# Attention tiles of a fused kernel: logits and turning of x in 64x64 blocks, tiles loaded in halves, weights loaded beside the first tiles

## The chip, the cores and the metric

The kernel runs on one core of one Trainium2 chip. Time is device microseconds (us) of one execution; three executions of the kernel before are shown below. Engines are TensorE (PE), VectorE (DVE), ScalarE (ACT), GpSimd (POOL) and SyncE (SP), which issues all the DMAs.

## The reference, cut to what matters

```python
# q, k, v: (8 batches, 8 heads, 576, 64)
scores = (q @ k.transpose(0, 1, 3, 2)) / sqrt(64)
Dmat[h] = where(i >= j, gamma[h] ** (i - j), 0)          # decay by distance
x = (scores * Dmat) @ v                                  # -> (4608 tokens, 512)
logits = x @ phi                                         # phi: 512 x 32 slots
d = exp(logits - logits.max(0)); d /= d.sum(0) + 1e-9    # over the tokens
slot_in = d.T @ x                                        # 32 x 512
slot_out[e] = relu(slot_in[e] @ w1[e]) @ w2[e]           # 8 experts, 4 slots each
c = exp(logits - logits.max(1)); c /= c.sum(1) + 1e-9    # over the slots
y = c @ slot_out
out = (((y @ fw1) * (y @ fw2)) @ fw3) @ w_out
```

## The kernel before

The 4608 tokens are 36 tiles of 128, in four groups of nine tiles (two batches each). Attention is computed by chunks of 64 positions with a running state: for each tile TensorE makes the scores inside the chunks (`scores`, L648), the products k and v that update the state (`update`, L661), the output through the states (`through_states`, L676) and through the masked scores (`through_scores`, L693, in two phases of 16 pairs). All of these are matmuls on 64x64 blocks of the array, four of which lie side by side. The result leaves in turned form (channels on the partitions); VectorE multiplies it by the decay and writes `x_t` (`scale_x`, L1249).

From `x_t` two things are made. `logits` (L711) multiplies by `phi` in the 128x32 shape, with `phi` as weights; the result, slots on the partitions, goes to the bank `RAW`, and ScalarE copies it to `logits_raw` (L1016). `turn_x` (L705) turns `x_t` by four 128x128 transposes into the bank `X_NAT`, and ScalarE copies it to `x_nat` (L1007). After each group VectorE and ScalarE compute maxima, exp and the combine weights `c_nat` (one step of it in each of the next tiles), and `dispatch` (L727, L732, 128x32 shape) sums exp times x over the group; ScalarE's `copy_sums` (L1050) takes the sum out of the same bank.

TensorE's order for tile n is written out in `step`: scores and update of n+1, a dispatch if one is due, logits of n-2, states of n, phase 0 of n, turn of n-1, phase 1 of n. TensorE runs it in a loop of nine passes with four steps as its body; parts that only some passes need (a dispatch, the logits of a tile before the first) stand in the body behind a branch. The other engines' orders are unrolled. In float32 one matmul of the program shows as two pairs of a weight load and a matmul.

SP issues everything from one queue, in a fixed order: the constants, tiles 0 and 1 in two halves each, tiles 2 and 3, weight unit 0, then tile by tile, with units 1 to 5 at tiles 4, 5 and 8 and four fold transfers behind tiles 10, 11, 14 and 15 (`FOLD_AT`). A tile is 1 MB with q turned, k turned, k, v; it is loaded when the tile four places before it is out (`out_ready`), as there are four places. A weight unit and a fold transfer are 1 MB too. POOL scales v as soon as the tile is there (`scale_v`, L561), and the scores of a tile wait for it (`v_ready`). Units 6 to 35 and two more folds wait for the last tiles or for the use of earlier units.

After the tiles TensorE makes the product of the last two weight matrices (`fold_part`, L794) in turns with the 36 expert and feature units (L809, L909), then pair features (L931) and the final product (L991).

Of the kernel before, what the change touches and what calls it, by code (L numbers as in the profile page):

```python
# [55 lines left out]
FOLD_AT = (10, 11, 14, 15)  # L56
# [24 lines left out]
def build(nc, pkg, consts, phi, units, fold_w, out, c_rows):  # L81
    ctx = ExitStack()
    with ctx:
# [39 lines left out]
        logits_raw = place("logits_raw", [P, 2, TILES * SLOTS])  # L123
# [101 lines left out]
        OUT_T, UPDATE, X_NAT, RAW = 2, 4, 6, 7  # L225
        STATE, LOGITS, MISC = 4, 6, 7

# [8 lines left out]
        tile_loaded = [sem(f"tile_loaded{i}") for i in range(SLOTS_IN)]  # L236
        first_loaded = [sem(f"first_loaded{i}") for i in range(2)]
# [10 lines left out]
        x_nat_ready = sem("x_nat_ready")  # L248
        logits_ready = sem("logits_ready")
# [6 lines left out]
        exp_ready = sem("exp_ready")  # L256
        raw_turned = sem("raw_turned")
        exp_nat_ready = sem("exp_nat_ready")
        sums_ready = sem("sums_ready")
        sums_copied = sem("sums_copied")  # L260
# [68 lines left out]
        def q_t(n):  # L329
            return tile_sb(n)[:, 0:D].rearrange("p (a n) -> p a n", a=PAIRS)  # L330

        def k_t(n):
            return tile_sb(n)[:, D:2 * D].rearrange("p (a n) -> p a n", a=PAIRS)

        def k_nat(n):
            return tile_sb(n)[:, 2 * D:3 * D]
# [101 lines left out]
        def _(sp):  # L438
            def load_tile(n):
# [16 lines left out]
            def load_first(t, half):  # L456

                lo, hi = 2 * D * half, 2 * D * (half + 1)
                sp.dma_start(pkg_sb[:, t, lo:hi], pkg[t].rearrange("(p c) -> p c", p=P)[:, lo:hi]
                             ).then_inc(tile_loaded[t] if half else first_loaded[t], 16)  # L460

            sp.dma_start(const_sb[:, 0:C_LATE], consts[:, 0:C_LATE]).then_inc(const_loaded, 16)
            for t in range(2):
                load_first(t, 1)
                load_first(t, 0)
# [4 lines left out]
            load_tile(2)  # L470
            load_tile(3)
# [17 lines left out]
            for u in range(6, UNITS):  # L489
# [3 lines left out]
                if u == 9:  # L493

                    sp.wait_ge(x_turned, NTILES)
# [143 lines left out]
        def _(pe):  # L639
# [44 lines left out]
            def through_scores(r, phase):  # L684

                for a in range(PAIRS):
                    for half in range(2):
# [10 lines left out]
                        elif phase == 1:  # L698
                            last.then_inc(phase_done, -1)
                        elif half == 0:  # L700
                            last.then_inc(x_t_ready if a == 0 else logits_copied, -1)

            def turn_x(r):
                for a in range(PAIRS):
                    last = nc.tensor.transpose(psum[:, X_NAT, P * a:P * (a + 1)], x_t[:, r % 2, a, :], ident)  # L705
                last.then_inc(x_turned, 1)

            def logits(r):
                for a in range(PAIRS):
                    for j in range(SUBS):  # L710
                        last = mm(psum[SLOTS * j:SLOTS * (j + 1), RAW, 0:SLOTS], phi_sb[:, a, :],  # L711
                                  x_t[:, r % 2, a, SLOTS * j:SLOTS * (j + 1)],
                                  start=(a == 0), stop=(a == PAIRS - 1))
                        if a == PAIRS - 1:
                            last.then_inc(logits_ready, 1)

            def dispatch(g):

                pe.wait_ge(exp_nat_ready, g + 1)
                pe.wait_ge(x_nat_ready, NTILES if g == GROUPS - 1 else dispatched_at(g) - 1)  # L720
# [20 lines left out]
            def step(i, r):  # L741
# [4 lines left out]
                else:  # L746
                    with pe.If(i < NTILES // SLOTS_IN - 1):
                        next_scores(after)
                for g in range(GROUPS - 1):
# [3 lines left out]
                if r > 1:  # L753
                    logits(two_before)
                else:
                    with pe.If(i > 0):
                        logits(two_before)

                pe.wait_ge(x_t_ready, 1)
                through_states(r)  # L760
                pe.wait_ge(logits_copied, 1)
                through_scores(r, 0)
                if r > 0:
                    turn_x(before)
                else:
                    with pe.If(i > 0):
                        turn_x(before)
# [3 lines left out]
            pe.wait_ge(first_loaded[0], 16)  # L771
# [3 lines left out]
            pe.wait_ge(first_loaded[1], 16)  # L775
# [78 lines left out]

            logits(SLOTS_IN - 2)
# [3 lines left out]
            logits(SLOTS_IN - 1)  # L859
            turn_x(SLOTS_IN - 1)  # L860
            fold(5)
# [20 lines left out]
            pe.wait_ge(x_nat_ready, NTILES)  # L882
# [119 lines left out]
        def _(act):  # L1002
            copy = nc.scalar.copy

            def copy_x(n):
                act.wait_ge(x_turned, n + 1)
                copy(x_nat[:, n % NAT_RING, :], psum[:, X_NAT, :]).then_inc(x_nat_ready, 1)  # L1007

            def copy_logits(n):
                g, t = divmod(n, TILES)  # L1010
                act.wait_ge(logits_ready, SUBS * (n + 1))
                if g >= 2 and t == 0:

                    act.wait_ge(raw_turned, g - 1)
                    act.wait_ge(exp_ready, g - 1)
# [561 lines left out]
```

## Time and profile before

| | us |
|---|---|
| median of 3 runs | 393.22 (392.13 to 396.33) |
| the profiled execution | 394.4 |
| its span, first to last instruction | 392.6 |
| TensorE matmuls busy | 358.9 (91%) |
| mean granted clock of TensorE | 0.969 |
| DMA | 104.77 MB, 267 GB/s over the span |

A row of a timeline begins with its start and its duration in us, then engine, line, operation, what it writes and reads, its shape and how many were merged; brackets give the engine's idle time before it and what ended that. TensorE's matmuls are pipelined: a group's duration reaches into the next group, so the time that a group takes is read from start to start.

### The profile page before, as it was taken

The page shows a single profiled execution, that of the slowest core. Times are in us where ns is not written, and L with a number is a line of the kernel's source. Part 1 is how long each engine was busy: PE and PEld are TensorE (multiplying, and loading weights), DVE is VectorE, ACT ScalarE, POOL GpSimd, SP SyncE. Part 2 cuts the span into 40 slices and gives each one's busy share as a digit, 9 for nine tenths or more (in the row PEclk, how much of TensorE's full clock was granted, in tenths as well). Part 3 has the DMA queues.
Part 4 walks back from the last instruction along what each step waited for, and adds up shares of the span by engine and source line. Part 5 has one row for each costly group of instructions (what it writes and reads, how often), then busy time and mean ns, then how long its engine had stood idle before and what let it go on. Part 6 is the DMA issues. An engine that isn't in the chain of part 4 may idle for free. (4 is left out here: it accounts for less than half of the span.)

```text
span 392.6 us, 16090 instructions
## 1 busy us (share of the span) xinstructions
PE 358.9 (91%) x7123; PEld 278.2 (71%) x7123; DVE 167.5 (43%) x329; ACT 125.2 (32%) x275; POOL 161.9 (41%) x155
## 2 busy tenths in 40 slices
PE   2683987898999999999999999899999999999996
PEld 1573876777878887774656555468878888888885
DVE  1321454556757765573013000699853323233320
ACT  1000121321433342222324220532734444434442
POOL 2521222322443542133546451298954554554530
PEclk9856799999999999999999999999999999999999
DMA  7898499897887886879999996057226655556222
GB/s 262 351 387 341 149 398 426 337 374 250 312 308 240 313 310 231 314 294 411 427 425 427 425 428 273 0 92 237 76 88 228 230 189 188 190 179 235 114 107 107
DMA packets 25914, 104.77 MB, mean 267 GB/s; under 512 B 2660, under 2 KB 5284, under 8 KB 16164
## 3 DMA queue, kind: packets, MB, share of 16 engines
q1 hardware_dynamic: 25892, 104.47, 71.1%
q8 instruction: 14, 0.23, 0.2%
q14 instruction: 8, 0.07, 0.0%
HBM read 94.14 MB, written 10.32 MB: 266 GB/s over the span
## 5 line engine op out<-in xcount | busy, mean ns | idle before, releaser
L561 POOL TENSOR_TENSOR pkg_sb<-pkg_sb,const_sb 128x512 f32<-128x512 f32 x36 | 37.5, 1042 | 106.4 <-DMA pkg_sb<-in_tiles 106.4
L623 POOL TENSOR_TENSOR feat<-c_sb 128x512 f32<-128x512 f32 x45 | 56.9, 1275 | 46.2 <-PE psum L991 44.3
L991 PE MATMUL psum<-m_hi,feat_hi 128*128 128x512 f32 x144 | 56.1, 390 | 0.3 <-DVE m_lo L1480 0.3
L991 PE MATMUL psum<-m_lo,feat_hi 128*128 128x512 f32 x144 | 56.0, 389 | 0.0
L991 PE MATMUL psum<-m_hi,feat_lo 128*128 128x512 f32 x144 | 56.0, 389 | 0.0
L428 DVE TENSOR_TENSOR feat_lo<-feat,feat_hi 128x512 fp32r<-128x512 f32 x34 | 27.2, 801 | 62.2 <-ACT feat_hi L1149 61.0
L1249 DVE TENSOR_TENSOR x_t<-psum,x_decay 128x512 f32<-128x512 f32 x36 | 24.9, 691 | 40.9 <-PE psum L693 40.9
L1007 ACT COPY x_nat<-psum 128x512 f32<-128x512 f32 x36 | 21.1, 586 | 65.8 <-PE psum L705 65.8
L648 PE MATMUL psum<-pkg_sb 64*64 64x64 f32 x1152 | 26.9, 234 | 16.2 <-POOL pkg_sb L561 7.3
L693 PE MATMUL psum<-weights_t,pkg_sb 64*64 64x64 f32 x1152 | 35.3, 238 | 5.7 <-issue 5.5
L1149 ACT CAST feat_hi<-feat 128x512 fp32r<-128x512 f32 x45 | 27.9, 623 | 39.0 <-POOL feat L623 39.0
L588 POOL TENSOR_TENSOR w_lo<-fold_raw,w_hi 128x512 fp32r<-128x512 f32 x14 | 18.2, 1298 | 45.1 <-ACT wo_hi L1066 45.0
L648 PEld LDWEIGHTS psum<-pkg_sb 64*64 64x64 f32 x1152 | 23.4, 146 | 17.7 <-issue 17.5
L693 PEld LDWEIGHTS psum<-weights_t,pkg_sb 64*64 64x64 f32 x1152 | 26.2, 141 | 12.9 <-issue 12.6
L991 PEld LDWEIGHTS psum<-m_hi,feat_hi 128*128 128x128 f32 x144 | 27.0, 188 | 6.2 <-issue 0.7
L1207 DVE TENSOR_TENSOR weights_t<-psum,const_sb 128x512 f32<-128x512 f32 x36 | 24.7, 686 | 15.6 <-PE psum L648 14.9
L991 PEld LDWEIGHTS psum<-m_hi,feat_lo 128*128 128x128 f32 x144 | 27.0, 188 | 5.6
L991 PEld LDWEIGHTS psum<-m_lo,feat_hi 128*128 128x128 f32 x144 | 27.0, 188 | 5.6
L1230 DVE TENSOR_TENSOR state_sb<-psum,state_sb 128x256 f32<-128x256 f32 x56 | 23.5, 420 | 14.7 <-PE psum L676 12.4
L676 PE MATMUL psum<-pkg_sb,state_sb 64*64 64x64 f32 x1152 | 26.7, 234 | 2.1 <-issue 1.6
L1193 ACT COPY out_sb<-psum 128x512 f32<-128x512 f32 x36 | 21.2, 589 | 21.5 <-PE psum L991 19.5
L661 PE MATMUL psum<-pkg_sb 64*64 64x64 f32 x1152 | 27.3, 234 | 0.7 <-issue 0.7
(138 smaller groups left out, 569.0 us busy)
## 6 DMA issues: line engine op xcount, KB each, us to landing
pkg_sb<-in_tiles SPq DMA_DIRECT2D x34, 1024.0 KB, 4.9
unit_a<-in_units SPq DMA_DIRECT2D x16, 1024.0 KB, 13.8
c_sb<-c_rows SPq DMA_DIRECT2D x45, 256.0 KB
unit_x<-in_units SPq DMA_DIRECT2D x9, 1024.0 KB, 14.1
out<-out_sb SPq DMA_DIRECT2D x36, 256.0 KB, 2.0
fold_raw<-in_fold SPq DMA_DIRECT2D x6, 1024.0 KB, 9.3
unit_y<-in_units SPq DMA_DIRECT2D x5, 1024.0 KB, 12.3
unit_n<-in_units SPq DMA_DIRECT2D x4, 1024.0 KB, 12.2
```

The source lines that it names most:

```text
L428: engine.tensor_tensor(feat_lo[:, k, :], feat[:, k, :], feat_hi[:, k, :].bitcast(F32), ALU.subtract).then_inc(done, 1)
L561: nc.gpsimd.tensor_tensor(v_nat(n).rearrange("p (h d) -> p h d", h=HEADS), v_nat(n).rearrange("p (h d) -> p h d", h=HEADS), decay.unsqueez ...
L623: nc.gpsimd.tensor_tensor(feat[:, k, :], c_sb[:, s, x, :], c_sb[:, s, y, :], ALU.mult).then_inc(feat_ready, 1)
L648: last = mm(psum[cols, odd, HD * a:HD * (a + 1)], k_t(r)[rows, a, cols], q_t(r)[rows, a, cols], start=True, stop=True)
L661: last = mm(psum[HD * odd:HD * (odd + 1), UPDATE + half, HD * a:HD * (a + 1)], k_nat(r)[rows, cols], v_nat(r)[rows, cols], start=True, sto ...
L676: last = mm(out_of(a, odd, half), state_sb[rows, (2 * r + half) % STATES_IN, a, :], q_t(r)[rows, a, HD * half:HD * (half + 1)], start=(hal ...
L693: last = mm(out_of(a, odd, half), v_nat(r)[rows, HD * h:HD * (h + 1)], weights_t[rows, r % 2, odd, HD * a:HD * (a + 1)], start=False, stop ...
L991: last = mm(psum[:, OUT + b, :], x, y, start=(at == 0 and m == 0), stop=(at == 4 and m == 2))
L1149: copy(feat_hi[:, ORDER[at], :], feat[:, ORDER[at], :]).then_inc(feat_hi_ready, 1)
L1207: tt(weights_t[:, n % 2, :, :].rearrange("p k (a n) -> p k a n", a=PAIRS), psum[:, 0:2, 0:D // 2].rearrange("p k (a n) -> p k a n", a=PAIR ...
L1230: tt(to, new, state_sb[:, c % STATES_IN, :, :].rearrange("p a n -> p (a n)"), ALU.add).then_inc(done, 1)
L1249: tt(x_t[:, n % 2, :, :].rearrange("p (k b) n -> p k (b n)", k=2), psum[:, OUT_T:OUT_T + 2, 0:D // 2], x_decay[:, :, n0:n0 + P].rearrange( ...
```

## The change

- `logits` becomes 16 matmuls on 64x64 blocks with `x_t` as weights and `phi` as the moving side: tokens come on the partitions, and the sum over the two halves of the channels comes in two parts, in two banks. ScalarE copies both parts (`logit_parts`); VectorE adds them once for tiles 0 to 7 of a group and once for tile 8 and transposes the sum into `logits_raw` (`add_parts`). The transpose that made `comb` is gone, as the sum already has that form.
- `turn_x` becomes 16 matmuls on 64x64 blocks with the identity as the moving side, in the same two banks as the logits. So logits wait for ScalarE's copy of x (`x_copied`), and the turn waits for the copy of the logits (`logits_copied`).
- `dispatch` moves behind the states of its step; a new semaphore, `dispatch_free`, tells that both banks are free; ScalarE copies the sums after the logits.
- A tile's layout is k turned, k, q turned, v; the first half is loaded once the scores and update of the tile four before are done, the second once that tile is out, and the keys of tile n+1 are issued ahead of q and v of tile n.
- Weight units 0 and 1 are issued behind tile 3, units 2, 3 and 4 at tile 4, unit 5 at tile 5; the four folds behind tiles 6, 7, 9 and 11.

```diff
-FOLD_AT = (10, 11, 14, 15)
+FOLD_AT = (6, 7, 9, 11)
-        OUT_T, UPDATE, X_NAT, RAW = 2, 4, 6, 7
+        OUT_T, UPDATE, X_NAT = 2, 4, 6
+        LOGITS_AT = D // 2
...
+            def load_keys(n):
+                if n >= SLOTS_IN:
+                    for i in range(2):
+                        sp.wait_ge(scores_ready[i], 2 * (n - SLOTS_IN + 1))
+                        sp.wait_ge(update_ready[i], 2 * (n - SLOTS_IN + 1))
+                sp.dma_start(tile_sb(n)[:, 0:2 * D], pkg[n].rearrange("(p c) -> p c", p=P)[:, 0:2 * D]
+                             ).then_inc(keys_loaded[place_of(n)], 16)
+            def load_q_v(n):
+                if n >= SLOTS_IN:
                     sp.wait_ge(out_ready, QUARTERS * (n - SLOTS_IN + 1))
-                sp.dma_start(tile_sb(n), pkg[n].rearrange("(p c) -> p c", p=P)).then_inc(tile_loaded[place_of(n)], 16)
+                sp.dma_start(tile_sb(n)[:, 2 * D:4 * D], pkg[n].rearrange("(p c) -> p c", p=P)[:, 2 * D:4 * D]
+                             ).then_inc(q_v_loaded[place_of(n)], 16)
...
+            for t in range(2, SLOTS_IN):
+                load_keys(t)
+                load_q_v(t)
             load_first_unit(0)
+            load_first_unit(1)
+            load_keys(SLOTS_IN)
             for n in range(SLOTS_IN, NTILES):
-                load_tile(n)
+                if n < NTILES - 1:
+                    load_keys(n + 1)
+                if n == SLOTS_IN:
+                    load_first_unit(2)
+                    load_first_unit(3)
+                load_q_v(n)
                 if n < SLOTS_IN + 2:
-                    load_first_unit(2 * n - 7)
-                    load_first_unit(2 * n - 6)
-                elif n == 8:
-                    load_first_unit(5)
+                    load_first_unit(n)
                 elif n in FOLD_AT:
...
             def scale_v(n):
-                pool.wait_ge(tile_loaded[place_of(n)], (n // SLOTS_IN + 1) * 16)
+                pool.wait_ge(q_v_loaded[place_of(n)], (n // SLOTS_IN + 1) * 16)
+                if n >= 2:
+                    pool.wait_ge(keys_loaded[place_of(n)], (n // SLOTS_IN + 1) * 16)
...
-            def turn_x(r):
+            def turn_x(r, consumes=True):
                 for a in range(PAIRS):
-                    last = nc.tensor.transpose(psum[:, X_NAT, P * a:P * (a + 1)], x_t[:, r % 2, a, :], ident)
-                last.then_inc(x_turned, 1)
+                    for odd in range(2):
+                        rows = slice(HD * odd, HD * (odd + 1))
+                        for half in range(2):
+                            cols = slice(HD * half, HD * (half + 1))
+                            last = mm(psum[cols, X_NAT + odd, HD * a:HD * (a + 1)], x_t[rows, r % 2, a, cols],
+                                      ident[rows, rows], start=True, stop=True)
+                            if (a, odd, half) == (0, 0, 0) and consumes:
+                                last.then_inc(logits_copied, -1)
+                            if a == PAIRS - 1:
+                                last.then_inc(x_turned, 1)
-            def logits(r):
+            def logits(r, consumes=True):
                 for a in range(PAIRS):
-                    for j in range(SUBS):
-                        last = mm(psum[SLOTS * j:SLOTS * (j + 1), RAW, 0:SLOTS], phi_sb[:, a, :],
-                                  x_t[:, r % 2, a, SLOTS * j:SLOTS * (j + 1)],
-                                  start=(a == 0), stop=(a == PAIRS - 1))
+                    for odd in range(2):
+                        rows = slice(HD * odd, HD * (odd + 1))
+                        for half in range(2):
+                            cols = slice(HD * half, HD * (half + 1))
+                            last = mm(psum[cols, X_NAT + odd, LOGITS_AT:LOGITS_AT + SLOTS], x_t[rows, r % 2, a, cols],
+                                      phi_sb[rows, a, :], start=(a == 0), stop=(a == PAIRS - 1))
...
+                if r > 1:
+                    pe.wait_ge(x_copied, 1)
+                    logits(two_before)
...
+                pe.wait_ge(x_t_ready, 1)
+                through_states(r)
                 for g in range(GROUPS - 1):
                     if dispatched_at(g) % SLOTS_IN == r:
                         with pe.If(i == dispatched_at(g) // SLOTS_IN):
                             dispatch(g)
...
                 through_scores(r, 0)
                 if r > 0:
+                    pe.wait_ge(logits_copied, 1)
                     turn_x(before)
...
+            def add_parts(g, last):
+                lo, hi = (SLOTS * (TILES - 1), SLOTS * TILES) if last else (0, SLOTS * (TILES - 1))
+                nat = comb[:, :, :].rearrange("p t s -> p (t s)")[:, lo:hi]
+                dve.wait_ge(group_copied, 2 * g + 1 + last)
+                if g > 0 and not last:
+                    dve.wait_ge(c_ready, g)
+                    dve.wait_ge(exp_ready, g)
+                tt(nat, logit_parts[:, 0, lo:hi], logit_parts[:, 1, lo:hi], ALU.add).then_inc(parts_added, 1)
+                dve.wait_ge(parts_added, 2 * g + 1 + last)
+                nc.vector.transpose(logits_raw[:, lo:hi], nat).then_inc(raw_turned, 1)
```

## Rows read from the trace of the kernel before

**Rows 1.** The page's 40 slices of 9.8 us: clock (tenths) and DMA rate.
```profile
PEclk9856799999999999999999999999999999999999
...
GB/s 262 351 387 341 149 398 426 337 374 250 312 308 240 313 310 231 314 294 411 427 425 427 425 428 273 0 92 237 76 88 228 230 189 188 190 179 235 114 107 107
```
**Rows 2.** Busy time by stretches: length, each engine, clock, DMA share, GB/s.
```profile
0.00:56.50 56.50, 36.71 (x1308) 32.16 (x1308) 18.18 (x35) 6.46 (x14) 13.83 (x18) 0.79 0.82 314
56.50:110.80 54.30, 46.83 (x2181) 40.16 (x2184) 31.26 (x64) 14.74 (x47) 15.62 (x15) 1.00 0.89 339
110.80:165.50 54.70, 53.70 (x2464) 45.17 (x2456) 35.70 (x76) 18.63 (x56) 19.75 (x18) 1.00 0.80 282
165.50:246.90 81.40, 81.40 (x574) 48.41 (x559) 16.88 (x40) 22.04 (x44) 33.45 (x26) 1.00 0.92 381
```
**Rows 3.** Timeline of VectorE: the products x_t of tiles 7, 20, 35.
```profile
56.51 0.69 DVE L1249 TENSOR_TENSOR x_t<-psum,x_decay 128x512 f32<-128x512 f32 x1 [1.08 <-PE psum L693]
...
110.83 0.69 DVE L1249 TENSOR_TENSOR x_t<-psum,x_decay 128x512 f32<-128x512 f32 x1 [1.11 <-PE psum L693]
...
165.49 0.69 DVE L1249 TENSOR_TENSOR x_t<-psum,x_decay 128x512 f32<-128x512 f32 x1 [1.89 <-PE psum L693]
```
**Rows 4.** Timeline of TensorE's matmuls: one step.
```profile
110.17 0.46 PE L693 MATMUL psum<-weights_t,pkg_sb 64*64 64x64 f32 x16
110.45 0.68 PE L648 MATMUL psum<-pkg_sb 64*64 64x64 f32 x32
110.91 0.68 PE L661 MATMUL psum<-pkg_sb 64*64 64x64 f32 x32
111.60 0.48 PE L711 MATMUL psum<-x_t,phi_sb 128*32 128x32 f32 x32
112.02 0.69 PE L676 MATMUL psum<-pkg_sb,state_sb 64*64 64x64 f32 x32
112.59 0.46 PE L693 MATMUL psum<-weights_t,pkg_sb 64*64 64x64 f32 x16
112.98 0.66 PE L705 MATMUL psum<-const_sb,x_t 128*128 128x128 f32 x4
113.56 0.46 PE L693 MATMUL psum<-weights_t,pkg_sb 64*64 64x64 f32 x16
```
**Rows 5.** Timeline of TensorE: nine transposes in a run.
```profile
251.72 1.15 PE L841 MATMUL psum<-const_sb,c_nat 128*128 128x128 f32 x9
```
**Rows 6.** Timeline of TensorE: a dispatch, and the group behind it.
```profile
114.93 1.92 PE L727 MATMUL psum<-x_nat,exp_nat 128*32 128x512 f32 x16
...
116.89 0.56 PE L711 MATMUL psum<-x_t,phi_sb 128*32 128x32 f32 x32
```
**Rows 7.** Timeline of TensorE: the loop's first pass, around its holes.
```profile
16.93 0.58 PE L693 MATMUL psum<-weights_t,pkg_sb 64*64 64x64 f32 x10 [2.98 <-issue]
...
32.94 0.34 PE L693 MATMUL psum<-weights_t,pkg_sb 64*64 64x64 f32 x8 [2.52 <-issue]
...
34.65 0.65 PE L711 MATMUL psum<-x_t,phi_sb 128*32 128x32 f32 x30
38.68 0.31 PE L711 MATMUL psum<-x_t,phi_sb 128*32 128x32 f32 x2 [3.39 <-issue]
```
**Rows 8.** The page's DMA queues: packets, MB, share.
```profile
q8 instruction: 14, 0.23, 0.2%
```
**Rows 9.** Who waited for whom, 56.5 to 110.8 us: total, times, longest.
```profile
PE psum L648 <- POOL pkg_sb L561: 7.3, 6, 1.5
```
**Rows 10.** The page's DMA issues: count, KB each, us to landing.
```profile
pkg_sb<-in_tiles SPq DMA_DIRECT2D x34, 1024.0 KB, 4.9
...
out<-out_sb SPq DMA_DIRECT2D x36, 256.0 KB, 2.0
```
**Rows 11.** Groups of instructions: count, busy us, mean ns, idle before, releaser.
```profile
L561 POOL TENSOR_TENSOR pkg_sb<-pkg_sb,const_sb 128x512 f32<-128x512 f32 x36 | 37.5, 1042 | 106.4 <-DMA pkg_sb<-in_tiles 106.4
...
L1007 ACT COPY x_nat<-psum 128x512 f32<-128x512 f32 x36 | 21.1, 586 | 65.8 <-PE psum L705 65.8
```

More of the change, by code:

```diff
@@ L235, in build @@
         fold_late_loaded = [sem(f"fold_late_loaded{j}") for j in range(FT // 4)]
-        tile_loaded = [sem(f"tile_loaded{i}") for i in range(SLOTS_IN)]
-        first_loaded = [sem(f"first_loaded{i}") for i in range(2)]
+        keys_loaded = [sem(f"keys_loaded{i}") for i in range(SLOTS_IN)]
+        q_v_loaded = [sem(f"q_v_loaded{i}") for i in range(SLOTS_IN)]
         v_ready = sem("v_ready")
@@ L699, in through_scores @@
                             last.then_inc(phase_done, -1)
-                        elif half == 0:
-                            last.then_inc(x_t_ready if a == 0 else logits_copied, -1)
-            def turn_x(r):
+                        elif (a, half) == (0, 0):
+                            last.then_inc(x_t_ready, -1)
+            def turn_x(r, consumes=True):
                 for a in range(PAIRS):
-                    last = nc.tensor.transpose(psum[:, X_NAT, P * a:P * (a + 1)], x_t[:, r % 2, a, :], ident)
-                last.then_inc(x_turned, 1)
@@ new lines, in logits @@
+            def logits(r, consumes=True):
+                for a in range(PAIRS):
+                    for odd in range(2):
[4 more added lines that the diff above has]
+                                      phi_sb[rows, a, :], start=(a == 0), stop=(a == PAIRS - 1))
+                            if (a, odd, half) == (0, 0, 0) and consumes:
+                                last.then_inc(x_copied, -1)
+                            if a == PAIRS - 1:
+                                last.then_inc(logits_ready, 1)
@@ L717, in dispatch @@
             def dispatch(g):
                 pe.wait_ge(exp_nat_ready, g + 1)
-                pe.wait_ge(x_nat_ready, NTILES if g == GROUPS - 1 else dispatched_at(g) - 1)
+                if g == GROUPS - 1:
+                    pe.wait_ge(x_nat_ready, 1)
+                else:
+                    pe.wait_ge(dispatch_free, g + 1)
                 def nat(t):
@@ L748, in step @@
                         next_scores(after)
+                if r > 1:
+                    pe.wait_ge(x_copied, 1)
+                    logits(two_before)
+                else:
+                    with pe.If(i > 0):
+                        pe.wait_ge(x_copied, 1)
+                        logits(two_before)
+                pe.wait_ge(x_t_ready, 1)
+                through_states(r)
                 for g in range(GROUPS - 1):
@@ L858, in _ @@
             pe.wait_ge(x_t_ready, 1)
-            logits(SLOTS_IN - 1)
+            logits(SLOTS_IN - 1, False)
+            fold(1)
+            pe.wait_ge(group_copied, 2 * GROUPS)
             turn_x(SLOTS_IN - 1)
-            fold(5)
+            fold(4)
             dispatch(GROUPS - 1)
@@ L1005, in copy_x @@
             def copy_x(n):
-                act.wait_ge(x_turned, n + 1)
-                copy(x_nat[:, n % NAT_RING, :], psum[:, X_NAT, :]).then_inc(x_nat_ready, 1)
+                act.wait_ge(x_turned, QUARTERS * (n + 1))
+                copy(x_nat[:, n % NAT_RING, :].rearrange("p (a k d) -> p k a d", a=PAIRS, k=2),
+                     psum[:, X_NAT:X_NAT + 2, 0:D // 2].rearrange("p k (a d) -> p k a d", a=PAIRS)
+                     ).then_inc(x_nat_ready if n == NTILES - 1 else x_copied, 1)
             def copy_logits(n):
@@ L1011, in copy_logits @@
                 act.wait_ge(logits_ready, SUBS * (n + 1))
-                if g >= 2 and t == 0:
-                    act.wait_ge(raw_turned, g - 1)
-                    act.wait_ge(exp_ready, g - 1)
-                copy(logits_raw[:, g % 2, SLOTS * t:SLOTS * (t + 1)], psum[:, RAW, 0:SLOTS]
-                     ).then_inc(group_copied if n == NTILES - 1 else logits_copied, 1)
-                if t == TILES - 1 and n < NTILES - 1:
+                if g > 0 and t in (0, TILES - 1):
+                    act.wait_ge(parts_added, 2 * g - (1 if t == 0 else 0))
+                copy(logit_parts[:, :, SLOTS * t:SLOTS * (t + 1)], psum[:, X_NAT:X_NAT + 2, LOGITS_AT:LOGITS_AT + SLOTS]
+                     ).then_inc(group_copied if n == NTILES - 1 else
+                                dispatch_free if n + 2 in [dispatched_at(i) for i in range(GROUPS - 1)] else
+                                logits_copied, 1)
+                if t >= TILES - 2 and n < NTILES - 1:
                     copy(mark[:, :], const_sb[0:1, 0:1]).then_inc(group_copied, 1)
@@ L1085, in relu_hidden @@
                                          ACT.Relu).then_inc(hid_ready, 1)
-            act.sem_inc(logits_copied, 2)
+            act.sem_inc(logits_copied, 1)
             for n in range(1, NTILES):
                 g, t = divmod(n, TILES)
-                if g > 0 and t == 7:
+                if g > 0 and t == 6:
                     exp_combine(g - 1)
+                if n > 1:
+                    copy_logits(n - 2)
                 if g > 0 and n == dispatched_at(g - 1):
                     copy_sums(g - 1)
-                if n > 1:
-                    copy_logits(n - 2)
                 copy_x(n - 1)
```

74 lines of the change are left out of this document (30 added, 44 removed).

## Prediction

> **What bounds the kernel now.** I read the page's slices first: in the first eighth the granted clock falls to 0.5, later it stays at full [rows 1]. So I cut the span by stages [rows 2]. Up to 165.5 us the 36 tiles of attention run; from there TensorE computes folds and expert units, idle nowhere up to 246.9 [rows 2], and then the final product. The change lies in the first stage. The rest is taken to move along unchanged: all 30 later weight units and two folds still wait for the last tiles, and TensorE has no hole behind them that earlier data could fill.
>
> Within the tile stage three parts have different limits; the marks are the products x_t of tiles 7, 20 and 35 [rows 3]. To 56.5 us TensorE is busy 36.7 us, and its longest holes are put down to "issue" [rows 2, 7]. From there to tile 20 it is idle 7.5 of 54.3 us, nearly all of it (7.3) behind the scaling of v, which itself waited for a transfer [rows 2, 9]. From tile 20 to 35 it is idle 1.0 of 54.7 us: the bare order of TensorE's work is the limit. Less two dispatches of 2.2 us (below) that is 50.3 / 15 = 3.36 us a tile.
>
> **Switching of shapes, steady tile.** A step of TensorE lasts 3.39 us, from one phase 1 (L693) to the next [rows 4]. The starts give its parts: phase 1 0.28, scores 0.46, update 0.69, logits (128x32) 0.42, states 0.57, phase 0 0.39, turn (128x128) 0.58. Scores, update and states are each 32 equal pairs of weight load and matmul in 64x64 shape, and 0.46 is what they take with no other shape beside them: update pays 0.23 and states 0.11 for the switch; phase 0, half as many pairs, pays 0.39 - 0.23 = 0.16. The new turn is 32 such pairs, 0.46 where four whole-width transposes and their switch took 0.58; a run of nine of those takes 1.15, some 0.11 each beside the 0.27 of the last [rows 5]. The new logits, 64x64 weights with 32 columns moving, are a form that no row has. They lie between 0.33 (now, less some 0.1 for the switch) and 0.46 (64 columns moving); I take 0.46, since their weights are as wide as those of scores. The step becomes 0.28 + 5 x 0.46 + 0.23 = 2.81: 0.58 less, or 0.71 at the lower end.
>
> **What comes near when a tile is that short.** Loads: a tile is issued when the tile four before is out, lands 4.9 us later, is scaled in 1.04 and some 0.15, and its output is ready 0.4 and two steps after that [rows 3, 10, 11]: 4.9 + 1.2 + 0.4 + 2 x 3.36 = 13.2 against 4 x 3.36 = 13.4. So whole loads are nearly late already, and at 2.81 they would be (12.1 against 11.2). For the half with q and v I interpolate between the 256 KB store (2.0) and the 1 MB load (4.9): 3.0, and 3.0 + 1.6 + 5.6 = 10.2 is in time. At the top end, 4.9, halving gains nothing. The keys' half goes out at its update; scale_v now waits for it too, but it had been sent a good half step earlier. SP is one queue in which the keys of n+1 stand ahead of q and v of n; their condition, update of n-3, is met early in the very step at whose end tile n-4 is out, so they hold nothing up. Bandwidth: 1 MB at the 426 GB/s of full slices is 2.46 us [rows 1], 88% of 2.81. The Trainium skill ("DMA: Bandwidth & Descriptors", Anatomy of one DMA) gives 2.0 us and bytes / 436e3 for a transfer on another issuing path and advises 1 MiB or more: 3.2 us for a half, an estimate. By it the loop would be 10.4, still in time.
>
> ScalarE: banks 6 and 7 now hold x and logits both, so logits wait for copy_x and the turn for copy_logits. A consumer starts 0.20 after the group that it waits for ends (110.83 against 110.17 + 0.46) [rows 3, 4]. From the turn's start 0.68 + 0.20 + 0.59 + 0.1 = 1.57 to the next logits, where TensorE arrives after 0.46 + 0.28 + 0.92 = 1.66; from logits to turn about 1.0 against 1.15 [rows 4, 11]. Behind copy_x ScalarE has four small moves and exp_t queued in one tile of nine; with exp_t taken as long as copy_x the turn waits some 0.4 there. VectorE gets one add and one transpose of 288 columns more a group, less the old transpose, each below the 0.69 of x_t's 512 [rows 3]: under 0.1 a tile, and it is busy 35.7 of 54.7 us [rows 2]. For all of this I allow 0.14 a tile: gain 0.44. Ends: 0 (the handshake takes all) and 0.71.
>
> **Dispatch.** It costs 116.89 - 114.93 = 1.96 us and some 0.2 for switches [rows 6]. It is moved behind states, between two 64x64 groups: one switch more (0.1 to 0.2). And copy_sums, a copy like copy_x (0.59), with 0.3 before and 0.1 behind it, now stands between it and the turn with phase 0 (0.23) as its only cover; before, logits, states and phase 0 hid it. I put 1.0 on each of three dispatches; between 0.2 and 1.5.
>
> **First pass of the loop.** There are five holes by "issue", of 2.98, 1.63, 0.72, 2.52 and 3.39 us, 11.2 in all ([rows 7]: the first and the last two). They lie evenly in the program. From the hole before 32.94 to that before 38.68 there are 8 + 30 pairs, 64 of scores and update between them, and 24 of a dispatch that is jumped over, 126; the others, counted from the start with 64 pairs ahead of the loop, stand at 218, 344, 470 and 596. The page has 14 transfers of the kind "instruction" with 0.23 MB, 16.4 KB each [rows 8]: this is code arriving, a block for each 126 pairs. The turn has 28 pairs more in each of four steps, so the body grows from 728 to 840 pairs and contains one block more. I add a mean hole, 2.2 (0.7 to 3.4). Against it stand eight shorter steps up to tile 7, near 0.5 each: -4. Units 1 to 5 and two folds move ahead into DMA time that is free there (share 0.82) [rows 2]. The second half of tile 4 is then queued behind units 2 and 3, up to 8 us later; its scores ran only behind the hole that ended at 32.94 [rows 7], so this costs 0, or 3 if the queue is longer. Sum -1.8.
>
> **Sum.** To tile 7: -1.8. To tile 20: 13 x -0.44 = -5.7, one dispatch +1.0, and of 7.5 us idle some 3.5 go, since only two folds (9 and 11) are still loaded between those tiles, where a unit and four folds of 2.46 us stood: -8.2. To tile 35: 15 x -0.44 + 2.0 = -4.6. Tail: the last group's add and turn for its last tile, two small operations with their waits, come into the chain from logits over exp_t to the last dispatch, whose cover of folds is used up already: +0.6. In all -14.0: the profiled run's 394.4 (span 392.6 and 1.8 around it) becomes 380.4; the median shown is 1.2 below that run, so 379.
>
> **Rivals.**
> A. Code that has to come back. At the loop's later returns no such hole is seen (TensorE idle 1.0 us over three of them) [rows 2]: the blocks up to pair 792, where the body ends (64 + 728), stay in place. Blocks end at pair 92, 218, ... 722, 848. So the body now reaches from the first block (64 is below 92) into the seventh; at 904 it enters the eighth. If the place for code is then full, the block fetched next displaces the one with the loop's head, and each of eight returns waits for code. Nothing hides that, so it costs at least the longest hole, 3.4: 27 us, of which the idle time behind transfers takes back 4. 380 + 23 = 403, and up to 418, as beside holes of that size the clock stood at 0.5 [rows 1, 7]. From 1.8 us a return on this decides for slower. For it: the even spacing, and that nothing shows more than seven blocks in use. Against it: no row shows that eight and one ahead are too many. The Trainium skill ("Runtime: NRT & Kernel Launch", Instruction fetch mechanics) says that TensorE keeps 128 KiB in blocks of 16 KiB, fetches the next block while it runs one, and stalls on a jump to a block that is gone. The size of a block agrees with the trace; 128 KiB are eight blocks, and a ninth would be fetched on entering the eighth. By that rule rival A comes true; no row of the kernel before shows it.
> A2. The same, but each refetch displaces the block needed next: eight blocks a pass at some 3 us instead of 1.9, above 430.
> B. The switch is not what costs the 0.58, or ScalarE's handshake takes its place. What is left is the loads' 3.5, less dispatches, the block and the tail: 387 to 396, little or no change.
>
> **How the numbers follow.** Forecast 0.47, with a range of its own of 372 to 387 (0.71 or 0.3 a tile, and the ends of the first pass); A 0.33; A2 0.07; B 0.11; anything else 0.02. The range of 370 to 412 takes in the forecast, B and most of A; A2 and A's top stay out. A measurement of this kernel can tell about 1%, 3.9 us, from no change. Faster than that: 0.47 and half of B, 0.52; within: 0.07; slower: 0.41.
>
> **What would show it.** Right: steps of 2.8 to 3.0 us between dispatches, 0.46 for update and for the turn; TensorE idle under 5 us from tile 7 to 20; six holes in the first pass and none of that size later. Wrong: holes of 3 us by "issue" at every fourth tile and more than 15 instruction transfers, or a clock below full after 60 us (A); turn or logits that wait for ScalarE's copies (B); scores that still wait for POOL's scaling (loads).

## The result, and the profile after

The changed kernel takes 555.8 us in the median of four runs (549.7 to 558.2), beside 392.7 for the kernel before: ratio 1.408, 95% interval 1.392 to 1.423. The forecast was 379, its range ended at 412. What came true is the mechanism of rival A2, which I had given 0.07, with nine blocks at each return of the loop instead of its eight.

The page of the changed kernel, TensorE's busy share by slices (13.9 us each here), its clock, DMA's rate, and the queue of code:
```profile
PE   3362553647546366553775589999999999999997
...
PEclk9665785967957778595777859999999999999999
...
GB/s 305 416 396 183 117 229 121 167 145 117 155 82 149 125 118 154 82 156 118 128 127 68 187 50 391 426 419 422 422 73 126 129 123 219 200 212 188 176 122 106
...
q8 instruction: 87, 1.43, 1.1%
```
Before, a clock below 0.8 ended with the first eighth [rows 1]; now it goes up and down until TensorE stands at 9 in every slice. The transfers of code are 87, where there were 14 [rows 8].

Stretches up to tiles 7, 20 and 35, and the folds and units behind them (columns as in [rows 2]), and the marks:
```profile
0.00:84.40 84.40, 40.06 (x1504) 37.25 (x1504) 18.36 (x36) 6.52 (x14) 15.71 (x19) 0.72 0.74 271
84.40:201.10 116.70, 62.05 (x2543) 56.32 (x2547) 33.59 (x72) 15.41 (x49) 16.32 (x15) 0.72 0.41 130
201.10:322.70 121.60, 69.79 (x2857) 61.61 (x2849) 37.15 (x78) 19.48 (x57) 17.46 (x16) 0.77 0.39 125
322.70:405.00 82.30, 82.04 (x589) 49.32 (x593) 17.40 (x42) 21.57 (x44) 33.42 (x26) 0.95 0.90 370
```
```profile
84.39 0.69 DVE L1291 TENSOR_TENSOR x_t<-psum,x_decay 128x512 f32<-128x512 f32 x1 [2.47 <-PE psum L710]
...
201.07 0.69 DVE L1291 TENSOR_TENSOR x_t<-psum,x_decay 128x512 f32<-128x512 f32 x1 [2.16 <-PE psum L710]
...
322.66 0.69 DVE L1291 TENSOR_TENSOR x_t<-psum,x_decay 128x512 f32<-128x512 f32 x1 [7.41 <-PE psum L710]
```
Against [rows 3] tile 7 is 27.9 us later; tiles 8 to 20 take 62.4 us more, tiles 21 to 35 66.9, and what follows 4.5 (554.3 - 322.66 against 392.6 - 165.49). So nearly all of it lies in the loop, 4.5 to 4.8 us a tile behind tile 7. From tile 7 on TensorE is idle 106.5 of 238.3 us (8.5 of 109.0 before, [rows 2]), and its own work takes 131.8 instead of 100.5, at a granted clock of 0.72 to 0.77 instead of 1.00. DMA's share there is 0.4, and no wait of TensorE behind tile 7 is put down to a transfer or to POOL's scaling: the loads no longer bound the loop.

Who is waited for, tile 7 to 35 (total, times, longest), and TensorE's matmuls behind holes by "issue" above 1.2 us in one pass of the loop, tiles 28 to 31:
```profile
PE psum L665 <- issue: 47.2, 14, 5.3
...
PE psum L710 <- issue: 29.6, 12, 4.2
...
PE psum L739 <- issue: 11.2, 8, 2.1
```
```profile
250.80 0.63 PE L678 MATMUL psum<-pkg_sb 64*64 64x64 f32 x28 [1.82 <-issue]
...
254.41 0.50 PE L710 MATMUL psum<-weights_t,pkg_sb 64*64 64x64 f32 x9 [1.63 <-issue]
...
260.04 1.12 PE L665 MATMUL psum<-pkg_sb 64*64 64x64 f32 x29 [3.85 <-issue]
...
262.99 0.37 PE L665 MATMUL psum<-pkg_sb 64*64 64x64 f32 x2 [1.84 <-issue]
...
275.24 0.33 PE L710 MATMUL psum<-weights_t,pkg_sb 64*64 64x64 f32 x2 [2.60 <-issue]
```
"Issue" with no releaser, in the middle of groups (29 of 32, 2 of 32, 9 of 16), is what the first pass of the kernel before showed where code arrived [rows 7]. The numbers fit: 87 transfers are 73 more than 14, and 73 = 8 x 9 + 1: one block more in the first pass, and nine at each of eight returns. The scores behind the longest hole take 1.12 for 29 pairs, where 32 take 0.68 in [rows 4].

### The profile page after: what moved, and what is told of

It is laid out like the page before. It is cut to its first block and busy times, and to the rows that moved or that the text cites. A ratio compares the mean times of both kernels' runs of the same rounds, so it can differ in the third digit from the quotient of the medians.

```text
span 554.3 us, 18299 instructions
## 1 busy us (share of the span) xinstructions
PE 398.0 (72%) x8131; PEld 319.0 (58%) x8131; DVE 172.6 (31%) x341; ACT 126.9 (23%) x279; POOL 162.0 (29%) x155
## 3 DMA queue, kind: packets, MB, share of 16 engines
q1 hardware_dynamic: 30788, 104.48, 52.6%
## 5 line engine op out<-in xcount | busy, mean ns | idle before, releaser
L665 PE MATMUL psum<-pkg_sb 64*64 64x64 f32 x1152 | 37.9, 272 | 65.0 <-issue 56.8
L710 PE MATMUL psum<-weights_t,pkg_sb 64*64 64x64 f32 x1152 | 47.9, 268 | 40.2 <-issue 39.8
L665 PEld LDWEIGHTS psum<-pkg_sb 64*64 64x64 f32 x1152 | 32.2, 179 | 67.8 <-issue 67.7
L710 PEld LDWEIGHTS psum<-weights_t,pkg_sb 64*64 64x64 f32 x1152 | 37.6, 173 | 45.3 <-issue 44.1
L693 PE MATMUL psum<-pkg_sb,state_sb 64*64 64x64 f32 x1152 | 38.1, 267 | 13.7 <-issue 13.6
L678 PE MATMUL psum<-pkg_sb 64*64 64x64 f32 x1152 | 35.9, 262 | 14.4 <-issue 14.4
L1056 ACT COPY logit_parts<-psum 128x64 f32<-128x64 f32 x36 | 7.7, 213 | 164.5 <-PE psum L739 164.5
L739 PE MATMUL psum<-phi_sb,x_t 64*64 64x32 f32 x1152 | 34.4, 251 | 13.5 <-issue 13.1
L693 PEld LDWEIGHTS psum<-pkg_sb,state_sb 64*64 64x64 f32 x1152 | 32.6, 176 | 15.3 <-issue 15.3
L739 PEld LDWEIGHTS psum<-phi_sb,x_t 64*64 64x64 f32 x1152 | 31.4, 176 | 15.3 <-issue 15.3
L678 PEld LDWEIGHTS psum<-pkg_sb 64*64 64x64 f32 x1152 | 31.3, 174 | 15.0 <-issue 15.0
L726 PE MATMUL psum<-const_sb,x_t 64*64 64x64 f32 x1152 | 34.2, 262 | 4.2 <-issue 2.9
```

The source lines that it names most:

```text
L665: last = mm(psum[cols, odd, HD * a:HD * (a + 1)], k_t(r)[rows, a, cols], q_t(r)[rows, a, cols], start=True, stop=True)
L678: last = mm(psum[HD * odd:HD * (odd + 1), UPDATE + half, HD * a:HD * (a + 1)], k_nat(r)[rows, cols], v_nat(r)[rows, cols], start=True, sto ...
L693: last = mm(out_of(a, odd, half), state_sb[rows, (2 * r + half) % STATES_IN, a, :], q_t(r)[rows, a, HD * half:HD * (half + 1)], start=(hal ...
L710: last = mm(out_of(a, odd, half), v_nat(r)[rows, HD * h:HD * (h + 1)], weights_t[rows, r % 2, odd, HD * a:HD * (a + 1)], start=False, stop ...
L726: last = mm(psum[cols, X_NAT + odd, HD * a:HD * (a + 1)], x_t[rows, r % 2, a, cols], ident[rows, rows], start=True, stop=True)
L739: last = mm(psum[cols, X_NAT + odd, LOGITS_AT:LOGITS_AT + SLOTS], x_t[rows, r % 2, a, cols], phi_sb[rows, a, :], start=(a == 0), stop=(a = ...
```

## The experiments

Two theories. *Code*: the body now reaches into an eighth block, the one behind it is fetched as well, and since the place for code doesn't hold nine, every pass fetches them all. *Work*: something in the new order (waits of the copies, the order of the loads, a clock kept low by them) makes the holes. The measure of position is [rows 7]'s: a block holds 126 pairs of weight load and matmul; blocks end at pair 92, 218 ... 848, 974; the body begins at 64; it ends at 792 before and at 904 after. The kernel before took 394.1, 392.4 and 392.7 in the three sets of runs; ratios are to it.

**Moving the loop without touching it.** 200 waits on the semaphore of the constants (they land at 2.7 us, ahead of the first tile, and from then on each wait is already met; 100 instructions, as many as 50 pairs) move the body from 64 to 114, behind the end of the first block; 80 of them move it only to 84.
```
             pe.wait_ge(keys_loaded[0], 16)      # changed kernel, ahead of the first scores
+            for _ in range(200):                # ahead40: range(80)
+                pe.wait_ge(const_loaded, 16)
```


> The changed kernel with 100 idle instructions (waits already met) on TensorE ahead of the loop, so that the loop's head moves out of the first block of code into the second and its end stays in the eighth. Theory of the code blocks (the loop with the block fetched ahead must fit eight blocks): no code comes back, under 25 instruction transfers instead of 87, and 375 to 388 us. Rival (the loads in halves and the early weights, or the handshake over the shared banks, make the kernel slow, and code comes late only because the queues are full): 545 to 560 us and some 87 transfers, as the work and its loads are the same.

> The same with 40 idle instructions: the loop's head stays in the first block. Theory of the code blocks: nothing is gained, 545 to 565 us and 85 to 90 instruction transfers. If a delay of the start by itself were what helps, it would lie between the changed kernel and the one with 100.

ahead100: 397.5 us, ratio 1.0125 (1.006 to 1.020), 16 code transfers. ahead40: 559.7, ratio 1.426 (1.415 to 1.438), 88 transfers. The same body, at 114 to 954, lies in seven blocks; at 84 to 924 in eight. Against the changed kernel 158 us are gone, by moving the loop 50 pairs. The count of transfers came out as expected, the time did not (375 to 388): what is left of the change is no faster than the kernel before. The waits themselves are dear:
```profile
13.66 1.13 PE L665 MATMUL psum<-pkg_sb 64*64 64x64 f32 x32 [13.66 <-issue]
```
The first scores ran at 6.66 before. So I moved it later by 25 matmuls in 64x64 shape (50 pairs) on a constant, into a bank that is not in use yet, while the first tile is still loading:
```
+            pe.wait_ge(const_loaded, 16)
+            for n in range(25):
+                at = HD * (n % 2)
+                mm(psum[at:at + HD, X_NAT + 1, 0:HD], const_sb[at:at + HD, C_MASK:C_MASK + HD],
+                   const_sb[at:at + HD, C_MASK:C_MASK + HD], start=True, stop=True)
```


> The changed kernel with the loop's head moved into the second block by 25 matmuls (100 instructions) ahead of the first scores, into a bank not yet in use, while TensorE waits for the first tile. They take little over 1 us where the 100 waits took 11. If only the late start made the kernel with 100 waits no faster than before: 388 to 392 us. If the loads take back what TensorE's steps gain whatever the start (their halves land 4.4 to 6 us after issue): 393 to 398.

394.0 us, ratio 1.0053 (1.0025 to 1.0082), 16 transfers. The first scores stand at 6.73, so the filler does not delay them; this is the change as it would be without its block, and it gains nothing: it is 0.5% slower than the kernel before.

**Making the loop of before longer with code that never runs.** Matmuls under a condition that is never met, 4 instructions each, are jumped over:
```
+                if r == 2:                      # kernel before, in the loop's body
+                    with pe.If(i > 5):
+                      with pe.If(i < 2):
+                        for _ in range(56):     # dead20: 20, dead35: 35
+                            mm(psum[0:HD, 0, 0:HD], k_t(r)[0:HD, 0, 0:HD], k_t(r)[0:HD, 0, 0:HD], start=True, stop=True)
```


> The kernel before with 80 instructions added in the middle of the loop's body that no pass ever runs; the body still ends in the seventh block. Theory of the code blocks: 391 to 396 us and 14 to 16 instruction transfers. Rival (a longer body costs by its length): a third of the loss, some 440.

> The kernel before with 140 such instructions, never run; the body now ends in the eighth block, its head is in the first. All work, all loads and their order are those of the kernel before. Theory of the code blocks: 85 to 90 instruction transfers and 530 to 570 us. Rival (the new shapes, halves or early weights are the cause): 391 to 396.

> The kernel before with 224 instructions in the loop's body that no pass runs, so that the body ends at the same place in the eighth block as that of the changed kernel (with 140 it ended some 40 instructions into that block, and code came back in only two of eight passes: 33 transfers, 421 to 442 us). Theory of the code blocks, made sharper by that run (the ninth block is asked for only some way into the eighth): code comes back in every pass, 80 to 90 transfers, 520 to 560 us, with all work and loads those of the kernel before. Rival (a body in eight blocks costs only now and then, and the changed kernel needs its other edits to be so slow): some 430.

dead20 ends the body at pair 832, in the seventh block: 393.7 us, ratio 1.0018 (0.998 to 1.006), 15 transfers; so the branches around the dead code cost at most about a microsecond. dead56 ends it at 904, where the change does: 552.2, ratio 1.409 (1.401 to 1.417). Its page, and its holes by "issue" above 1.2 us between 248 and 284 us:
```profile
PEclk9655875777767798567766679999999999999999
...
q8 instruction: 87, 1.43, 1.1%
```
```profile
251.51 0.51 PE L676 MATMUL psum<-pkg_sb,state_sb 64*64 64x64 f32 x19 [1.53 <-issue]
...
257.77 1.12 PE L648 MATMUL psum<-pkg_sb 64*64 64x64 f32 x29 [4.49 <-issue]
...
260.82 0.37 PE L648 MATMUL psum<-pkg_sb 64*64 64x64 f32 x2 [1.93 <-issue]
...
268.86 0.26 PE L711 MATMUL psum<-x_t,phi_sb 128*32 128x32 f32 x4 [1.24 <-issue]
...
277.96 0.66 PE L711 MATMUL psum<-x_t,phi_sb 128*32 128x32 f32 x32 [3.27 <-issue]
```
All work, loads and waits are those of the kernel before, yet time, clock (0.826 and 0.840 in the mean) and count of transfers are the changed kernel's. This settles it: where the body ends, as counted in blocks from its head, is the whole 160 us, the low clock included. dead35 ends it at 862, only 14 pairs into the eighth block: its two runs took 421.1 and 442.4, not the 530 to 570 expected, and the profiled one (442.4) has 33 transfers, 19 more than 14, which is 2 x 9 + 1. Behind 60 us its holes by "issue" above 1 us stand in two stretches alone, 132 to 162 and 184 to 206 us; the first of each:
```profile
132.36 1.12 PE L648 MATMUL psum<-pkg_sb 64*64 64x64 f32 x29 [5.43 <-issue]
...
184.15 1.12 PE L648 MATMUL psum<-pkg_sb 64*64 64x64 f32 x29 [4.76 <-issue]
```
So code came back in two passes of eight. That in these the block behind was asked for before the loop returned, and in the others not, is my reading; no row shows the request. The edge is where [rows 7]'s spacing put it.

**Fewer, wider instructions.** If only the switch between a full-width shape and 64x64 were dear, the new matmuls could be merged in twos (64 rows by 128 columns of weights), and the body would fit without a filler.
```
-   for half in range(2):                                      # logits; the turn likewise
-       cols = slice(HD * half, HD * (half + 1))
-       mm(psum[cols, X_NAT + odd, LOGITS_AT:...], x_t[rows, r % 2, a, cols], phi_sb[rows, a, :], ...)
+   mm(psum[:, X_NAT + odd, LOGITS_AT:...], x_t[rows, r % 2, a, :], phi_sb[rows, a, :], ...)
```


> The changed kernel with logits and turn as 8 matmuls each of 64 rows by 128 columns of the array instead of 16 of 64x64: 16 pairs each, so the body shrinks to 712 pairs and ends in the seventh block with nothing put ahead. Theory of the code blocks: under 20 transfers and no code that comes back, 385 to 400 us. Of the shape switch: four switches a step are back, so a step lasts 3.1 to 3.4 us instead of 2.97, and turn and logits some 0.1 us more each; if the switch costs nothing, a step stays at 3.0 or falls, as each has half the pairs.

435.4 us in the median of four runs (422.7 to 435.9), 14 transfers: no code comes back, as expected, but the time is far above the 385 to 400 expected. One step, at a granted clock of 1.00:
```profile
120.84 1.08 PE L735 MATMUL psum<-phi_sb,x_t 64*128 64x32 f32 x16
121.85 0.69 PE L693 MATMUL psum<-pkg_sb,state_sb 64*64 64x64 f32 x32
122.36 0.41 PE L710 MATMUL psum<-weights_t,pkg_sb 64*64 64x64 f32 x16
122.71 1.11 PE L724 MATMUL psum<-const_sb,x_t 64*128 64x64 f32 x16
123.75 0.46 PE L710 MATMUL psum<-weights_t,pkg_sb 64*64 64x64 f32 x16
```
Logits take 1.01 and the turn 1.04 from start to start, for 16 pairs, twice what 32 pairs of 64x64 take (0.45 and 0.49, below). From tile 20 to 35 wide takes 70.1 us, m_shapes (below) 52.6. The half-wide shape is no way round the code.

**Which part of the rest gains, which loses.** loads_only is the kernel before with the loads of the change alone (halves, early weights). Three kernels with the filler divide the change: m_shapes has the 64x64 shapes alone, with whole loads and weights in the old order; m_whole adds the early weights; aheadmm has the halves too.
```
-    load_keys(n + 1) ... load_q_v(n)          # m_shapes, m_whole: a tile is one transfer again,
+    load_tile(n)                              # sent when the tile four before is out
-FOLD_AT = (6, 7, 9, 11)                       # m_shapes alone: units 1 to 5 and the folds in the old order
+FOLD_AT = (10, 11, 14, 15)
```


> The kernel before with the changed loads alone: tiles in two halves, keys first, units and folds beside the first tiles. The body is that of before, so no code comes back. If the loads by themselves gain (tiles 8 to 20 no longer wait for 1 MB behind folds): 386 to 390 us. If halves cost what the early weights gain: 391 to 396.

> The same, and the weights load beside the first tiles as in the change. Theory 1: the early weights alone put tile 7 some 3 us later and the middle tiles get half of it back: 391 to 393 us. Theory 2: no difference beyond 1 us from whole loads with late weights.

> The 64x64 logits and turns alone, with the 25 matmuls ahead of the loop that keep its body out of the eighth block; tiles are loaded whole again, and weights where they were. Theory 1 (shorter steps are real, a gain of 0.31 us each as in the run with the 100 waits, and the halves and the early weights took them back): tile 35 near 162.5, 3 earlier than before, and 390 to 391 us. Theory 2 (the lesser gain goes to the dispatches and the scaling of v, halves or not): tile 35 at 165 and 393 to 395 us.

| kernel | median us | ratio (95%) | tile 7 | tile 20 | tile 35 |
|---|---|---|---|---|---|
| before | 392.7 | 1 | 56.5 | 110.8 | 165.5 |
| loads_only | 392.4 | 1.0012 (0.998 to 1.004) | 58.6 | 107.9 | 162.8 |
| m_shapes | 389.5 | 0.9935 (0.990 to 0.997) | 54.8 | 105.7 | 158.4 |
| m_whole | 391.3 | 0.9984 (0.996 to 1.001) | 61.1 | 107.9 | 160.9 |
| aheadmm | 394.0 | 1.0053 (1.003 to 1.008) | 62.2 | 111.5 | 165.0 |

The marks are of single executions, the medians of ten or more. m_shapes is the one version here (but for those below that leave loads out) that beats the kernel before, by 3.3 us in the medians; its profiled run was 5.7 ahead in span, as the one of before, 394.4, lies 1.7 above that kernel's median and its own, 388.7, 0.8 below. On top of the new shapes the early weights take 1.8 back and the halves 2.7 more. On the kernel before, both together cost nothing (loads_only); why they cost something only beside the new shapes stays open. In aheadmm a half of 512 KB lands after 5.5 us, a whole tile in m_shapes after 4.8:
```profile
pkg_sb<-in_tiles SPq DMA_DIRECT2D x72, 512.0 KB, 5.5
```
```profile
pkg_sb<-in_tiles SPq DMA_DIRECT2D x34, 1024.0 KB, 4.8
```
and TensorE's scores wait for the scaling of v (which waits for the transfer) between tiles 7 and 20, first in aheadmm, then in m_whole, then in m_shapes:
```profile
PE psum L665 <- POOL pkg_sb L578: 5.0, 5, 2.0
```
```profile
PE psum L665 <- POOL pkg_sb L578: 3.0, 4, 1.7
```
```profile
PE psum L664 <- POOL pkg_sb L577: 5.9, 5, 1.9
```
So in these tiles the early weights save 2.9 us of waits and the halves take 2.0 of them back. What the early weights cost lies ahead of tile 7, where m_whole is 6.3 later than m_shapes; its granted clock was 0.72 there against 0.97, but aheadmm, at 1.00, is as late.

One step and a dispatch of m_shapes (scores L664, update L677, logits L738, states L692, phases L709, turn L725, dispatch L759 and L764):
```profile
105.06 0.44 PE L709 MATMUL psum<-weights_t,pkg_sb 64*64 64x64 f32 x16
105.29 0.68 PE L664 MATMUL psum<-pkg_sb 64*64 64x64 f32 x30
...
105.83 0.67 PE L677 MATMUL psum<-pkg_sb 64*64 64x64 f32 x30
106.33 0.67 PE L738 MATMUL psum<-phi_sb,x_t 64*64 64x32 f32 x32
106.78 0.70 PE L692 MATMUL psum<-pkg_sb,state_sb 64*64 64x64 f32 x32
107.34 0.52 PE L709 MATMUL psum<-weights_t,pkg_sb 64*64 64x64 f32 x16
107.73 0.69 PE L725 MATMUL psum<-const_sb,x_t 64*64 64x64 f32 x32
108.22 0.44 PE L709 MATMUL psum<-weights_t,pkg_sb 64*64 64x64 f32 x16
...
110.56 1.92 PE L759 MATMUL psum<-x_nat,exp_nat 128*32 128x512 f32 x16
112.27 0.43 PE L764 MATMUL psum<-x_nat,exp_nat 128*32 128x128 f32 x8
112.63 0.46 PE L709 MATMUL psum<-weights_t,pkg_sb 64*64 64x64 f32 x16
113.54 0.70 PE L725 MATMUL psum<-const_sb,x_t 64*64 64x64 f32 x32 [0.46 <-ACT group_sum L1096]
```
The step is 108.22 - 105.06 = 3.16 against 3.39 [rows 4]. Over the plain steps between tiles 20 and 35 (eleven each; those with a dispatch are left out) the starts give these means, before and here: scores 0.47 and 0.48, update 0.63 and 0.52, logits 0.40 and 0.45, states 0.55 and 0.55, phase 0 0.39 and 0.32, turn 0.59 and 0.48, phase 1 0.37 and 0.38. The whole step goes from 3.40 to 3.18, 0.22 less.

**With loads that bound nothing.** From tile 4 on only the quarter of the tile with v is loaded; q and both forms of k stay those of tiles 0 to 3, so the result is of other data.
```
+                lo = 0 if n < SLOTS_IN else 3 * D
-                sp.dma_start(tile_sb(n), pkg[n].rearrange("(p c) -> p c", p=P))...
+                sp.dma_start(tile_sb(n)[:, lo:4 * D], pkg[n].rearrange("(p c) -> p c", p=P)[:, lo:4 * D])...
```


> The kernel before, with the same edit of the loads: steps of 3.3 from tile 4 on, tile 35 near 158, 384 to 387 us. If tiles 4 to 7 are no faster than in the kernel before, their holes were not the loads'.

> The 64x64 kernel with whole loads and late weights, where from tile 4 on only the quarter with v is loaded (q and both forms of k stay those of tiles 0 to 3, so the result is of other data): loads bound nothing. Theory 1: steps of 3.0 from tile 4 on, tile 35 near 148; against the same edit on the kernel before it is 0.3 a tile shorter, some 9 us less 2 for the dispatches: 7 us. Theory of the prediction (0.44 to 0.58 a tile): 12 to 16 us.

thin_before 384.5 us (383.7 to 386.1), thin_mm (the same on m_shapes) 382.6 (381.5 to 383.7). TensorE's waits for the scaling of v between tiles 4 and 20 are down to 0.6 and 1.4 us. Tiles 20 and 35, first of thin_before, then of thin_mm:
```profile
100.84 0.69 DVE L1251 TENSOR_TENSOR x_t<-psum,x_decay 128x512 f32<-128x512 f32 x1 [1.11 <-PE psum L695]
...
155.56 0.69 DVE L1251 TENSOR_TENSOR x_t<-psum,x_decay 128x512 f32<-128x512 f32 x1 [1.89 <-PE psum L695]
```
```profile
101.28 0.69 DVE L1297 TENSOR_TENSOR x_t<-psum,x_decay 128x512 f32<-128x512 f32 x1 [0.88 <-PE psum L711]
...
153.37 0.69 DVE L1297 TENSOR_TENSOR x_t<-psum,x_decay 128x512 f32<-128x512 f32 x1 [1.76 <-PE psum L711]
```
Without the loads the shapes gain 2.6 us in 15 tiles, where I had expected 7 us in all and measured 1.9: thin_mm is 3.0 behind at tile 4 (46.9 against 43.8), still 2.6 behind at tile 7, gains 2.2 from there to tile 20 and 2.6 from 20 to 35, and gives 1.5 back after tile 35 (228.5 against 227.0 to the end). The loads cost the kernel before about 8 us.

## Why the prediction was wrong, step by step

- **The step that failed is the price of the eighth block.** The sum had it as "one block more", a mean hole of 2.2 us, once, in the first pass; for the later passes it put nothing, though no row showed that an eighth block has a place of its own. It measured 20.4 us at each of eight returns, (555.8 - 392.7) / 8, or 2.3 us for each of nine blocks. In the seven returns from tile 7 to 35 these are 18.5 us each: 14.0 more idle time of TensorE ((106.5 - 8.5) / 7) and 4.5 more of its own work at the lower clock ((131.8 - 100.5) / 7).
- **Rival A had the place right and the price wrong too.** The edge at pair 848, the body that counts from 64 and the fetch ahead of need all held (ahead100, ahead40, dead20, dead56). But A said that "the block fetched next displaces the one with the loop's head", one hole of 3.4 us at each return, 27 us; 73 transfers more are nine a return, not one. If each block that arrives displaces the one needed soonest, a loop that runs through its blocks in a fixed order finds every one of them gone; I had this as A2 and gave it 0.07, though nothing in the rows spoke for one displaced block rather than all. Which block is displaced is inferred from the count; no row shows it.
- **The Trainium skill** ("Runtime: NRT & Kernel Launch", Instruction fetch mechanics), which I had cited for eight blocks held and the next fetched ahead, is borne out in this by the runs: seven blocks and the one behind stay (14 to 16 transfers), eight and the one behind don't (87 and 88). The same section also speaks of only two blocks held and of crossings that are mostly hidden. The runs decide against both: a loop over seven blocks refetches none, and the first pass waits at each crossing, 0.4 to 4.4 us in m_shapes.
- **What "would show it"** held: more than 15 instruction transfers, holes by "issue", a clock below full after 60 us. Not one hole of 3 us at every fourth tile, but a row of them from 1.2 to 5.3 through the pass.
- **The switch, 0.44 a step.** With the block out of the way (m_shapes, tiles 21 to 35) the 13 tiles without a dispatch take 40.9 us instead of 43.7, 0.22 each. I had put every 64x64 group at 0.46, and so 0.23 on the update's switch, 0.11 on that of states, 0.16 on phase 0's and 0.12 on the turn's. They gave 0.11, 0.01, 0.07 and 0.11; the turn alone was right. The one step that I read [rows 4] had one of the longest updates (0.69; the mean is 0.63), and states take 0.55 with no other shape beside them, so their excess was not the switch. Rival B was half true: most of the 0.58 was not the switch; a wait for ScalarE's copies shows in the dispatch steps alone.
- **Dispatch, +1.0.** The two dispatch steps of that stretch grew from 5.46 to 5.86 while a plain one shrank by 0.22: 0.6 each. The wait that I named is there, 0.46 for copy_sums.
- **First pass, -1.8.** m_shapes gives -1.7, and six holes by "issue", as forecast (1.53, 1.99, 3.77, 0.72, 4.40 and 0.40 us). But dead20, with the shapes and loads of before, has its tile 7 at 54.8 as well; both ran that stretch at a granted clock of 0.97, the kernel before at 0.79 [rows 2]. So the -1.7 does not show that the shapes gained it. The price of the early weights, 0 to 3 us, was wrong: at tile 7 m_whole is 6.3 later than m_shapes. The half transfers, put at 3.0 us by interpolation between a store and a whole load, took 5.5: which lies outside the range of its rows (2.0 to 4.9). That the keys' half, sent early, delays the half that is needed fits this; no run shows it by itself.
- **Tiles 8 to 20, -8.2, and 21 to 35, -4.6.** aheadmm: -5.0 and -1.1; m_shapes: -3.4 and -2.0. **Tail, +0.6**: 1.4 in m_shapes (386.9 - 158.35 = 228.5 against 227.1).
- So without the block the change as a whole comes out at 394 (aheadmm), within 1% of before, where the sum said 379: of the 15 us missing, 7.5 are the first pass, 6.7 the steps and the waits for transfers behind it, 0.8 the tail.

## What to carry to other kernels

Before an unrolled loop is made longer, count its instructions and the blocks that they touch, from where the loop starts: in this kernel a block within the place for it cost one hole, of 4.4 us at most in m_shapes, in the first pass; one block too many cost all blocks at every pass. The first pass's holes by "issue" and the transfers of the kind "instruction" give the spacing for this, and a filler ahead of the loop or dead code in it tells in one run whether the edge is the cause. And a cost of some tenths that is read from one step, as the switch of shapes was here, should be a mean over all steps of the stretch: the one that I read was among the longest.

## What the runs showed of the hardware that was not expected

- Eight blocks of code where seven fit, with one fetched ahead: 14 transfers become 87, 393 us become 552 with the same work (dead56), and 14 pairs into the eighth block it happens in two passes of eight (33 transfers).
- Where holes of a few microseconds return through the whole loop the granted clock is lower: 0.72 to 0.77 in that of the changed kernel, 0.73 to 0.74 in dead56's, 0.97 to 1.00 in that of m_shapes. A few of them don't settle it: up to tile 7 m_whole had 0.72 and aheadmm 1.00, each with holes by "issue" of up to 4 us.
- Waits that are already met are not free: 200 of them put the first scores at 13.66 instead of 6.66 us, some 11 us behind the constants, while 25 matmuls in the same place (3.0 us of TensorE's time) put them at 6.73.
- 64x128 weights cost 0.065 us a pair, 64x64 weights 0.015 (1.04 / 16 against 0.49 / 32), so merging two quarters doubles the time instead of halving it.
